# Expert stage of a token-routing kernel: row numbers made ahead of the new pick, X two steps sooner

## The chip, the cores and the metric

One NeuronCore of one Trainium2 chip runs the whole program in one launch. The metric is the device time of one execution in microseconds, smaller is better. The engines are TensorE (PE, with its weight loads as PEld), VectorE (DVE), ScalarE (ACT), GpSimd (POOL) and SyncE (SP); each runs its own list of instructions in order and waits on semaphores for the others.

## The reference

Three layers follow each other: a linear attention with decay, a dense feed-forward layer, and a mixture of 8 experts with a fixed capacity. The change concerns the last alone.

```python
def _attn_ref(r, k, v, w, u):                 # 4 batches, 8 heads, 768 steps, 48 features
    for t in range(S):
        y[:, :, t] = einsum('bhd,bhde->bhe', rt, state + (u * kt) outer vt)
        state = wt[:, :, :, None] * state + kt outer vt

def _moe_ref(x, w_in, w_out):                 # 3072 x 384, 384 x 2048, 2048 x 384
    h = x @ w_in
    return (h * np.tanh(softplus(h))) @ w_out

def _moe2_ref(x, w_gate, w1, w2):             # 8 experts, each 384 x 1024 and 1024 x 384
    cap = N // E                              # 384 tokens for each expert
    for idx in np.argsort(-(x @ w_gate).flatten()):
        tok, e = int(idx) // E, int(idx) % E  # best pair first; skip taken tokens, full experts
        ...
    for e in range(E):
        out[assigned == e] = np.maximum(x[assigned == e] @ w1[e], 0.0) @ w2[e]
```

## The kernel before

The first stage (attention and dense layer) runs over 12 blocks of 256 tokens. Its end leaves 3072 rows of 384 numbers in DRAM (`x2_d`) and the scores `L` of 24 x 8 for each of the 128 partitions in SBUF.

The second stage has to find out which 384 tokens go to which expert. It does so in rounds r = 0 to 6, called searches here: each names the expert that fills up first and the threshold above which its tokens lie, by six steps of a search with 32 thresholds at once. One step is: VectorE compares all keys with the 32 limits (`cmp`), TensorE counts in 24 small matmuls (`counts`), VectorE marks which experts are full (`filled`), TensorE sums the marks over the limits in one small matmul (`maxima`), VectorE makes the next limits (`next_step`). After the sixth step VectorE chooses expert and members (`choose`), TensorE makes their running numbers (`ranks`), VectorE takes the chosen tokens out and picks each remaining token's best expert anew (`pick_expert`, `one_hot_expert`, `start_search`).

The running numbers have to become a list of token numbers by slot: VectorE splits each number into digits and makes one-hot rows of them (`digits`, `numbered`, `one_hot_low`), TensorE multiplies them (unit I), VectorE masks the result (`id_blocks`), TensorE spreads it (unit J), VectorE sums it to `ids` (`token_ids`). With `ids` GpSimd gathers the expert's rows from DRAM (`rows_in`).

The expert's own work on TensorE is cut into units. X is nine transposes of the gathered rows, whose result ScalarE rounds to fp16 (`xgT_hi`) and VectorE reduces to a remainder (`low_xg`). H0 to H7 are nine matmuls each of 384 columns with the first weights; ScalarE rounds each, VectorE makes its remainder (`low_h`). Y0 to Y7 are nine matmuls each with the second weights, added up in three banks. H0 waits for both parts of X; Yf waits for both parts of Hf. After Y7, ScalarE copies the rows out of the banks.

TensorE's list is written out by hand. In every search there are 13 places for units, written in `PLACES`: place A of step t lies between `counts` and `maxima` of that step, place B behind `maxima`, and place C behind `ranks`. `units(r, where, do)` says which expert is meant; expert p is the one that search p chose. Before, I, J, X, H0 to H3 and Y0 of search r belong to expert r-1, the others to expert r-2. VectorE's list is written out in the loop over searches, with `low_h` and `low_xg` put between the search's own instructions. While nothing is there for TensorE in search 1, products that nobody reads are run (`idle_products`). Behind the last search the same places go on without counts and maxima until expert 7 is done.

Of the kernel before, what the change touches and what calls it, by code (L numbers as in the profile page):

```python
# [14 lines left out]
B, H, S, D = 4, 8, 768, 48  # L15
# [7 lines left out]
NT = N // P  # L23
# [37 lines left out]
def moe_chain(nc, wt_d, kt_d, rt_d, r_d, k_d, v_d, u_d, win_d, wout_d, wg_d, wot_d, w1_d, w2_d, out_d):  # L61
# [4 lines left out]
    with ctx:  # L66
# [223 lines left out]
        def split_out(n):  # L290
# [4 lines left out]

        PLACES = {("A", 0): ["Y1"], ("B", 0): ["H4"], ("A", 1): ["I", "Y2"], ("B", 1): ["J", "H5"],
# [3 lines left out]
        YOUNG = ("X", "H0", "H1", "H2", "Y0", "H3")  # L300
        ORDER = [(c, t) for t in range(NSTEP) for c in "AB"] + [("C", 0)]
# [4 lines left out]
        def units(r, where, do):  # L306
            for u in PLACES[where]:
                p = r - 1 if u in YOUNG + ("I", "J") else r - 2
                if 0 <= p < E:
                    do(p, u[0], int(u[1:] or 0))  # L310
# [112 lines left out]
        def _(pe):  # L423
# [358 lines left out]
            for r in range(E - 1):  # L782
                if r == 1:
                    idle_products(16)
                for t in range(NSTEP):
                    counts(r, t)
                    units(r, ("A", t), unit)
                    if r == 0:
                        sums(NI - 1, SUMS["B", t], slice(0, 3))
                    maxima(r, t)  # L790
                    if r == 1 and t < 4:
                        idle_products(6)
                    units(r, ("B", t), unit)
                    if r == 0:
                        sums(NI - 1, SUMS["B", t], slice(3, None))
                ranks(r)
                units(r, ("C", 0), unit)
            ranks(E - 1)
# [193 lines left out]
        def _(dve):  # L992
# [135 lines left out]

            def pick_expert(js=slice(0, NT), fill_a=None, fill_b=None):
                n = js.stop - js.start  # L1130
                link(V.tensor_reduce(val[:, js], L3[:, js, :], AX.X, ALU.max))
                if fill_a:
                    fill_a()
                link(V.tensor_tensor(less[:, js, :], L3[:, js, :], over_e(val[:, js]), ALU.is_lt))
                link(V.tensor_tensor(tmp3[:, js, :], less[:, js, :], over_j(eighths[:, :], n), ALU.add))
                if fill_b:
                    fill_b()
                link(V.tensor_reduce(pick[:, js], tmp3[:, js, :], AX.X, ALU.min))
# [301 lines left out]
            for t in range(2, NSTEP):  # L1440
                link(V.tensor_scalar(grid[t][:, :], iota_t[:, :], wid[:, t:t + 1], None, ALU.mult))

            for r in range(E - 1):
                new, old = r - 1, r - 2
                if r >= 1:
                    one_hot_low()
                filled(r, 0)
                low_h(old, 3)
                next_step(r, 0)
                filled(r, 1)  # L1450
                if r >= 1:
                    id_blocks(r - 1)
                low_h(old, 4)
                next_step(r, 1)
                if r >= 1:
                    token_ids(r - 1)
                filled(r, 2)
                low_h(old, 5)
                next_step(r, 2)
                filled(r, 3)  # L1460
                low_h(old, 6)
                next_step(r, 3)
                filled(r, 4)
                low_h(old, 7)
                next_step(r, 4)
                low_xg(new)
                filled(r, 5)
                choose(r)
                pick_expert(slice(0, NT), lambda: low_h(new, 0), lambda: low_h(new, 1))
                if r < E - 2:  # L1470
                    one_hot_expert()
                else:
                    weight_row(E - 1, pick[:, 0:1])
                take_slots(r)
                leave()
                if r < E - 2:
                    start_search()
                    digits()
                    numbered()
                    low_h(new, 2)  # L1480
            did(V.memset(mem[:, NT:2 * NT], 0.0))
            link(V.tensor_scalar(mem[:, 0:NT], gone[:, :], 0.0, None, ALU.is_equal))
            prefixes()
            low_h(E - 3, 2)
            digits()
            numbered()
            low_h(E - 3, 3)
            one_hot_low()
            low_h(E - 3, 4)
            id_blocks(E - 2)  # L1490
            token_ids(E - 2)
            low_h(E - 3, 5)
            take_slots(E - 1)
            digits()
            numbered()
            low_h(E - 3, 6)
            one_hot_low()
            low_h(E - 3, 7)
            low_xg(E - 2)
            for f in range(6):  # L1500
                low_h(E - 2, f)
                if f == 4:
                    id_blocks(E - 1)
                    token_ids(E - 1)
            low_h(E - 2, 6)
# [181 lines left out]
```

## Time and profile before

| what | value |
|---|---|
| median of 3 runs | 799.06 us (798.05 to 803.17) |
| the profiled execution | 798.34 us, its span 796.6 us |
| first stage, about | 0 to 513 us |
| searches 0 and 1, about | 513 to 565 us |
| searches 2 to 6 | 565 to 720.7 us |
| what follows search 6 | 720.7 to 796.6 us |
| busy over the span | PE 97%, PEld 72%, DVE 79%, ACT 53%, POOL 37% |

The profile is of one execution; its time is told beside its span, and 1.74 us lie outside the span. Times in the rows below are microseconds from the start of the span. "start us, us" are start and length of an instruction or of a row of equal ones (x24 is 24 of them); what stands in brackets is how long the engine was idle before it and who released it. A row of matmuls is pipelined, so that the next one may begin up to 0.16 us before the printed end. In a row of windows the bounds and the length come first, then the busy us of each engine with its number of instructions (PE, PEld, DVE, ACT, POOL, or PE alone), the granted clock of TensorE as a share of 2.4 GHz, the busy share of the DMA engines and GB/s.

### The profile page before, as it was taken

What the parts mean: (1) busy time and instruction counts of PE and PEld (TensorE: products, weight loads), DVE (VectorE), ACT (ScalarE), POOL (GpSimd) and SP (SyncE); (2) the same over time, 40 slices, a digit from 0 to 9 for tenths busy, and PEclk for the clock granted to TensorE, in tenths of its full rate; (3) what the DMA queues carried; (4) which work ended last, traced back from release to release, by engine and by line L of the source; (5) the groups of instructions that cost most, each with busy time, mean ns of one, the idle gap of its engine ahead of it and who ended that gap; (6) DMA issues with size and microseconds to landing.
All of it is one profiled execution on the core that took longest, in us unless ns stands there. A gap on an engine that the chain in (4) does not pass through costs nothing.

```text
span 796.6 us, 17145 instructions
## 1 busy us (share of the span) xinstructions
PE 769.7 (97%) x6810; PEld 577.1 (72%) x6810; DVE 628.6 (79%) x1081; ACT 425.1 (53%) x703; POOL 292.7 (37%) x244
## 2 busy tenths in 40 slices
PE   8899999999999999999999999987999999999994
PEld 8888878787878787878787877655565665666662
DVE  8969999999998999998999985877776767766220
ACT  2478759595968595868686779410121221222221
POOL 4424482627272727272726350011221231222311
PEclk9999999999999999999999999995999999999998
DMA  9962266464656464655464347114423415415500
GB/s 306 377 210 64 78 201 245 144 237 142 233 187 213 151 230 159 212 210 196 170 208 174 117 154 248 61 53 157 172 90 148 188 61 189 187 44 207 218 31 30
DMA packets 47791, 133.49 MB, mean 168 GB/s; under 512 B 5344, under 2 KB 19808, under 8 KB 45664
## 3 DMA queue, kind: packets, MB, share of 16 engines
q1 hardware_dynamic: 38880, 93.07, 33.7%
q0 software_dynamic: 5376, 34.61, 11.8%
q10 hardware_dynamic: 3456, 4.72, 1.7%
q8 instruction: 54, 0.88, 0.4%
q14 instruction: 25, 0.20, 0.1%
HBM read 97.78 MB, written 34.60 MB: 166 GB/s over the span
## 4 chain that ended last, share of the span: by engine, by line
PE 83%; DVE 10%; issue 2%; DMA 2%; ACT 2%; POOL 0%; SPq 0%; DVEq 0%
PE bank L425 80%; DVE cmp L1316 2%; DMA stage<-in_moe_w_out 1%; DVE g_lo L1416 1%; ACT t_sb L807 1%; PE bank L730 1%; PE bank L450 1%; PE bank L511 1%; DVE inv L1008 1%; DMA k_tok<-in_k 1%; DVE t_sb L1395 1%; DVE rdec L1023 0%; DVE t_sb L1388 0%; DVE t_sb L1391 0%; DVE thr L1333 0%
## 5 line engine op out<-in xcount | busy, mean ns | idle before, releaser
L425 PE MATMUL bank<-x_hi,win_hi 128*128 128x256 f16 (+1 forms) x588 | 158.8, 272 | 1.6 <-DVE h_sb L1080 0.9
L425 PE MATMUL bank<-x_lo,win_hi 128*128 128x256 f16 (+1 forms) x588 | 158.7, 272 | 0.0
L425 PE MATMUL bank<-x_hi,win_lo 128*128 128x256 f16 (+1 forms) x588 | 158.7, 272 | 0.0
L1547 POOL TENSOR_TENSOR g_lo<-t_sb,g_hi 128x512 f16<-128x512 f32 x88 | 122.3, 1420 | 47.0 <-ACT g_hi L807 47.0
L425 PE MATMUL bank<-wout_hi,g_hi 128*128 128x392 f16 (+1 forms) x416 | 129.0, 317 | 0.0
L425 PE MATMUL bank<-wout_lo,g_hi 128*128 128x392 f16 (+1 forms) x416 | 128.8, 316 | 0.0
L425 PE MATMUL bank<-wout_hi,g_lo 128*128 128x392 f16 (+1 forms) x416 | 128.7, 316 | 0.0
L807 ACT ACTIVATE g_lo<-bank 128x384 f16<-128x384 f32 x64 | 31.4, 490 | 144.1 <-PE bank L425 124.7
L1530 POOL TENSOR_TENSOR dv<-v_tok,dot 128x384 f32<-128x384 f32 x24 | 29.8, 1240 | 186.7 <-DVE dot L1038 186.7
L807 ACT ACTIVATE g_hi<-t_sb 128x512 f16<-128x512 f32 x96 | 56.5, 624 | 54.6 <-PE bank L425 54.4
L1087 DVE TENSOR_TENSOR t_sb<-t_sb,h_sb 128x512 f32<-128x512 f32 x96 | 83.0, 913 | 2.0 <-ACT t_sb L807 1.4
L1008 DVE RECIPROCAL inv<-cum 128x256 f32<-128x256 f32 x48 | 82.1, 1733 | 0.7
L807 ACT ACTIVATE t_sb<-h_sb 128x512 f32<-128x512 f32 x96 | 59.8, 623 | 37.5 <-DVE h_sb L1080 37.5
L807 ACT ACTIVATE t_sb<-t_sb,half 128x512 f32<-128x512 f32 x96 | 68.6, 715 | 0.1
L425 PEld LDWEIGHTS bank<-x_hi,win_hi 128*128 128x128 f16 x588 | 61.0, 104 | 9.7 <-issue 1.0
L1416 DVE SCALAR_TENSOR_TENSOR g_lo<-bank,g_lo 128x384 f16<-128x384 f32 x64 | 35.1, 549 | 40.5 <-ACT g_lo L807 34.1
L425 PEld LDWEIGHTS bank<-x_hi,win_lo 128*128 128x128 f16 x588 | 60.9, 104 | 6.0
L425 PEld LDWEIGHTS bank<-x_lo,win_hi 128*128 128x128 f16 x588 | 59.2, 101 | 6.3
L807 ACT ACTIVATE h_sb<-bank 128x512 f32<-128x512 f32 (+1 forms) x72 | 38.5, 556 | 43.4 <-PE bank L425 41.6
L807 ACT ACTIVATE t_sb<-t_sb,half_pi 128x512 f32<-128x512 f32 x96 | 60.8, 710 | 0.1
L1633 POOL DMA_INDIRECT out<-h_sb,ids x24 | 23.6, 983 | 98.1 <-ACT h_sb L807 93.3
L425 PEld LDWEIGHTS bank<-wout_hi,g_lo 128*128 128x128 f16 x416 | 42.9, 105 | 22.6
(184 smaller groups left out, 1593.7 us busy)
## 6 DMA issues: line engine op xcount, KB each, us to landing
stage<-in_moe_w SPq DMA_DIRECT2D x22, 768.0 KB, 6.5
w_split<-stage SPq DMA_DIRECT2D x22, 768.0 KB, 4.5
fold_w<-in_moe_w SPq DMA_DIRECT2D x10, 768.0 KB, 8.9
w_split<-fold_w SPq DMA_DIRECT2D x10, 768.0 KB, 7.6
wt<-in_w_turned SPq DMA_DIRECT2D x24, 258.0 KB, 2.8
kt<-in_k_turned SPq DMA_DIRECT2D x24, 256.0 KB, 2.6
rt<-in_r_turned SPq DMA_DIRECT2D x24, 256.0 KB, 2.8
r_tok<-in_r SPq DMA_DIRECT2D x24, 192.0 KB, 6.0
```

Of the source, the lines that this page charges most:

```text
L425: return nc.tensor.matmul(*a, **k)
L450: last = nc.tensor.transpose(T2[:, q * P:(q + 1) * P], kdiv[n % CH][:, q, :], ident[:, :])
L511: last = nc.tensor.transpose(Y[:, k3 * P:(k3 + 1) * P], x_tok[c][:, k3 * P:(k3 + 1) * P], ident[:, :])
L730: last = nc.tensor.transpose(bank[3 + k3][:, m * P:(m + 1) * P], xg[m][:, k3 * P:(k3 + 1) * P], ident[:, :])
L807: return nc.scalar.activation(out, in_, f, **k)
L1008: V.reciprocal(inv[:, qs, :], cum[n % CH][:, qs, 1:PW]).then_inc(s["inv"], 1)
L1087: V.tensor_tensor(t, t, h_sb[:, j * GW:(j + 1) * GW], ALU.mult).then_inc(s["g"], 1)
L1316: V.tensor_tensor(cmp[:, :, :], over_t(x[:, :], NTHR), limits[:, :].rearrange("p (o i) -> p o i", o=1).to_broadcast([P, NT, NTHR]), ALU.is ...
L1416: V.scalar_tensor_tensor(h_lo[f % 3][:, :], bank[3 + f % 3][:, 0:CAP], 0.0, h_hi[f % 3][:, :], ALU.max, ALU.subtract).then_inc(s["hlo"], 1)
L1530: G.tensor_tensor(dv[:, :, :], v_tok[c][:, :, :], dot[:, :].rearrange("p (h o) -> p h o", o=1).to_broadcast([P, H, D]), ALU.mult).then_inc ...
L1547: G.tensor_tensor(g_lo[:, j * GW:(j + 1) * GW], t_sb[:, j * GW:(j + 1) * GW], g_hi[:, j * GW:(j + 1) * GW], ALU.subtract).then_inc(s["glo" ...
L1633: G.indirect_dma_start(out_d, bass.IndirectOffsetOnAxis(ap=ids[p % 3][:, m:m + 1], axis=0), y_sb[m][:, :], None).then_inc(s["yout"], 16)
```

## The change

`PLACES` is written anew. X stands two steps earlier (place B of step 2 instead of step 4). Places A of steps 2 and 3 are empty, H0 and H1 follow in B of step 3, and from there one unit stands in each place until C, which holds seven: H4, Y2, I, H5, J, Y3, H6. I and J there are of the expert that this very search has chosen. Only Y4, H7, Y5, Y6 and Y7 are left for the next search.

VectorE's list follows. After `choose` it makes the row numbers at once (`take_slots`, `digits`, `numbered`, `one_hot_low`, `id_blocks`), and only then the new pick, and `token_ids` ahead of `start_search`. `low_xg` moves from behind step 4's `next_step` to behind step 2's. The idle products of search 1 move: 28 now stand behind `ranks` of search 0, around I and J of expert 0, and 12 in search 1 (before 40 in search 1). The number and the shape of all other instructions stay as they are.

```diff
--- before.py
+++ after.py
@@ -293,11 +293,11 @@
 
 
 
-        PLACES = {("A", 0): ["Y1"], ("B", 0): ["H4"], ("A", 1): ["I", "Y2"], ("B", 1): ["J", "H5"],
-                  ("A", 2): ["Y3"], ("B", 2): ["H6"], ("A", 3): ["Y4"], ("B", 3): ["H7"],
-                  ("A", 4): ["Y5"], ("B", 4): ["X", "Y6"], ("A", 5): ["Y7"],
-                  ("B", 5): ["H0", "H1"], ("C", 0): ["H2", "Y0", "H3"]}
-        YOUNG = ("X", "H0", "H1", "H2", "Y0", "H3")
+        PLACES = {("A", 0): ["Y4"], ("B", 0): ["H7", "Y5"], ("A", 1): ["Y6"], ("B", 1): ["Y7"],
+                  ("A", 2): [], ("B", 2): ["X"], ("A", 3): [], ("B", 3): ["H0", "H1"],
+                  ("A", 4): ["Y0"], ("B", 4): ["H2"], ("A", 5): ["Y1"], ("B", 5): ["H3"],
+                  ("C", 0): ["H4", "Y2", "I", "H5", "J", "Y3", "H6"]}
+        OLDER = ("Y4", "H7", "Y5", "Y6", "Y7")
         ORDER = [(c, t) for t in range(NSTEP) for c in "AB"] + [("C", 0)]
 
 
@@ -305,7 +305,7 @@
 
         def units(r, where, do):
             for u in PLACES[where]:
-                p = r - 1 if u in YOUNG + ("I", "J") else r - 2
+                p = r - 2 if u in OLDER else r if u in ("I", "J") else r - 1
                 if 0 <= p < E:
                     do(p, u[0], int(u[1:] or 0))
 
@@ -780,21 +780,26 @@
                     mm(bank[2][:, 0:TOK], x_hi[0][:, 0, 0:P], x_hi[0][:, 1, :], start=True, stop=True)
 
             for r in range(E - 1):
-                if r == 1:
-                    idle_products(16)
                 for t in range(NSTEP):
                     counts(r, t)
                     units(r, ("A", t), unit)
                     if r == 0:
                         sums(NI - 1, SUMS["B", t], slice(0, 3))
                     maxima(r, t)
-                    if r == 1 and t < 4:
+                    if r == 1 and t < 2:
                         idle_products(6)
                     units(r, ("B", t), unit)
                     if r == 0:
                         sums(NI - 1, SUMS["B", t], slice(3, None))
                 ranks(r)
-                units(r, ("C", 0), unit)
+                if r == 0:
+                    idle_products(8)
+                    unit(0, "I", 0)
+                    idle_products(8)
+                    unit(0, "J", 0)
+                    idle_products(12)
+                else:
+                    units(r, ("C", 0), unit)
             ranks(E - 1)
             for r in range(E - 1, E + 2):
                 for where in ORDER:
@@ -1126,15 +1131,11 @@
             def over_t(x, n):
                 return x.rearrange("p (j o) -> p j o", o=1).to_broadcast([P, NT, n])
 
-            def pick_expert(js=slice(0, NT), fill_a=None, fill_b=None):
+            def pick_expert(js=slice(0, NT)):
                 n = js.stop - js.start
                 link(V.tensor_reduce(val[:, js], L3[:, js, :], AX.X, ALU.max))
-                if fill_a:
-                    fill_a()
                 link(V.tensor_tensor(less[:, js, :], L3[:, js, :], over_e(val[:, js]), ALU.is_lt))
                 link(V.tensor_tensor(tmp3[:, js, :], less[:, js, :], over_j(eighths[:, :], n), ALU.add))
-                if fill_b:
-                    fill_b()
                 link(V.tensor_reduce(pick[:, js], tmp3[:, js, :], AX.X, ALU.min))
 
             def one_hot_expert(js=slice(0, NT)):
@@ -1440,68 +1441,61 @@
             for t in range(2, NSTEP):
                 link(V.tensor_scalar(grid[t][:, :], iota_t[:, :], wid[:, t:t + 1], None, ALU.mult))
 
+            def steps_of(r):
+
+                filled(r, 0)
+                next_step(r, 0)
+                low_h(r - 2, 7)
+                filled(r, 1)
+                next_step(r, 1)
+                filled(r, 2)
+                next_step(r, 2)
+                low_xg(r - 1)
+                filled(r, 3)
+                next_step(r, 3)
+                low_h(r - 1, 0)
+                filled(r, 4)
+                low_h(r - 1, 1)
+                next_step(r, 4)
+                filled(r, 5)
+                low_h(r - 1, 2)
+                choose(r)
+
+            def row_numbers():
+                digits()
+                numbered()
+                one_hot_low()
+
             for r in range(E - 1):
-                new, old = r - 1, r - 2
-                if r >= 1:
-                    one_hot_low()
-                filled(r, 0)
-                low_h(old, 3)
-                next_step(r, 0)
-                filled(r, 1)
-                if r >= 1:
-                    id_blocks(r - 1)
-                low_h(old, 4)
-                next_step(r, 1)
-                if r >= 1:
-                    token_ids(r - 1)
-                filled(r, 2)
-                low_h(old, 5)
-                next_step(r, 2)
-                filled(r, 3)
-                low_h(old, 6)
-                next_step(r, 3)
-                filled(r, 4)
-                low_h(old, 7)
-                next_step(r, 4)
-                low_xg(new)
-                filled(r, 5)
-                choose(r)
-                pick_expert(slice(0, NT), lambda: low_h(new, 0), lambda: low_h(new, 1))
+                steps_of(r)
+                low_h(r - 1, 3)
+                take_slots(r)
+                row_numbers()
+                low_h(r - 1, 4)
+                id_blocks(r)
+                pick_expert(slice(0, NT))
                 if r < E - 2:
                     one_hot_expert()
                 else:
                     weight_row(E - 1, pick[:, 0:1])
-                take_slots(r)
+                token_ids(r)
                 leave()
                 if r < E - 2:
                     start_search()
-                    digits()
-                    numbered()
-                    low_h(new, 2)
+                low_h(r - 1, 5)
+                low_h(r - 1, 6)
             did(V.memset(mem[:, NT:2 * NT], 0.0))
             link(V.tensor_scalar(mem[:, 0:NT], gone[:, :], 0.0, None, ALU.is_equal))
             prefixes()
-            low_h(E - 3, 2)
-            digits()
-            numbered()
-            low_h(E - 3, 3)
-            one_hot_low()
-            low_h(E - 3, 4)
-            id_blocks(E - 2)
-            token_ids(E - 2)
-            low_h(E - 3, 5)
             take_slots(E - 1)
-            digits()
-            numbered()
-            low_h(E - 3, 6)
-            one_hot_low()
             low_h(E - 3, 7)
+            row_numbers()
             low_xg(E - 2)
-            for f in range(6):
+            for f in range(5):
                 low_h(E - 2, f)
-                if f == 4:
-                    id_blocks(E - 1)
-                    token_ids(E - 1)
+            id_blocks(E - 1)
+            low_h(E - 2, 5)
+            token_ids(E - 1)
             low_h(E - 2, 6)
             low_h(E - 2, 7)
             low_xg(E - 1)
```

## Rows read from the trace of the kernel before

**Rows 1.** The page: span and chain that ended last, by engine.

```profile
span 796.6 us, 17145 instructions
...
PE 83%; DVE 10%; issue 2%; DMA 2%; ACT 2%; POOL 0%; SPq 0%; DVEq 0%
```

**Rows 2.** Windows: the whole of search 3 (busy us of each engine, clock, DMA).

```profile
595.96:627.16 31.20, 30.92 (x313) 18.85 (x312) 22.87 (x73) 6.43 (x14) 7.76 (x8) 1.00 0.38 139
```

**Rows 3.** Timeline of TensorE, two steps of search 5 (start us, length us).

```profile
666.83 0.76 PE L425 MATMUL bank<-oh,cmp 128*32 128x8 bf16 x24
...
669.09 0.17 PE L425 MATMUL bank<-full,rest_b 32*128 32x8 bf16 x1
...
670.80 0.76 PE L425 MATMUL bank<-oh,cmp 128*32 128x8 bf16 x24
```

**Rows 4.** Timeline of TensorE: three units of expert 6, one more, and the last products.

```profile
737.96 4.55 PE L425 MATMUL bank<-g_hi,win_hi 128*128 128x384 f16 x27
...
742.35 1.63 PE L425 MATMUL bank<-win_lo,g_lo 128*128 128x384 f16 x9
...
782.96 4.55 PE L425 MATMUL bank<-wout_lo,g_lo 128*128 128x384 f16 x27 [1.27 <-DVE g_lo L1416]
```

**Rows 5.** Timelines of TensorE, ScalarE and VectorE, one X in search 4.

```profile
645.83 0.17 PE L425 MATMUL bank<-full,rest_b 32*128 32x8 bf16 x1
...
646.58 1.25 ACT L807 ACTIVATE g_hi<-bank 128x384 f16<-128x384 f32 x3 [2.45 <-PE bank L730]
...
647.64 1.48 DVE L1424 SCALAR_TENSOR_TENSOR g_hi<-bank,g_hi 128x384 f16<-128x384 f32 x3
...
649.32 0.15 DVE L1326 TENSOR_SCALAR full<-bank 32x8 bf16<-32x8 f32 x1 [0.20 <-PE bank L425]
```

**Rows 6.** Timelines of TensorE and VectorE, end of search 0.

```profile
530.13 0.17 PE L425 MATMUL bank<-full,ones_b 32*128 32x8 bf16 x1
...
532.17 0.26 DVE L1354 TENSOR_TENSOR_SCAN before<-mem,zeros 128x47 bf16<-128x47 bf16 x1
...
533.10 0.35 DVE L1131 TENSOR_REDUCE val<-L 128x24 f32<-128x192 f32 x1
...
536.49 0.17 DVE L1384 TENSOR_SCALAR high<-slot 128x24 f32<-128x24 f32 x1
...
537.78 0.95 DVE L1395 TENSOR_TENSOR t_sb<-low,iota_lo 128x768 f16<-128x768 f32 x1
```

**Rows 7.** Timelines of TensorE and GpSimd, search 1 and the start of search 2.

```profile
536.72 0.74 PE L425 MATMUL bank<-oh,cmp 128*32 128x8 bf16 x24 [2.27 <-DVE cmp L1316]
...
540.57 0.80 PE L425 MATMUL bank<-oh,cmp 128*32 128x8 bf16 x24 [0.78 <-DVE cmp L1316]
...
543.41 0.80 PE L425 MATMUL bank<-oh,cmp 128*32 128x8 bf16 x24
...
544.56 0.18 PE L425 MATMUL bank<-full,rest_b 32*128 32x8 bf16 x1 [0.35 <-DVE full L1326]
...
547.36 0.95 POOL L1626 DMA_INDIRECT h_sb<-x_rows,ids  x1 [0.30 <-issue]
...
551.72 2.18 PE L730 MATMUL bank<-ident,h_sb 128*128 128x128 f32 x9
...
555.25 5.51 PE L425 MATMUL bank<-g_hi,win_hi 128*128 128x384 f16 x18
...
565.13 0.76 PE L425 MATMUL bank<-oh,cmp 128*32 128x8 bf16 x24
```

**Rows 8.** Windows: TensorE and its granted clock where it falls and rises.

```profile
71.20:74.90 3.70, 2.79 (x27) 1.00 0.21 69
...
75.50:76.00 0.50, 0.50 (x5) 0.50 0.96 299
...
534.46:539.00 4.54, 0.89 (x26) 1.00 0.77 271
...
555.20:560.60 5.40, 5.40 (x19) 2.62 (x20) 4.00 (x17) 0.49 (x1) 2.02 (x2) 0.54 0.19 41
```

## The prediction

> **What bounds the kernel now.** I read the chain that ended last first. It is TensorE's for 83% of the span [rows 1], so a wait of another engine counts only where TensorE stands still for it. Then the windows, one for each search: TensorE is busy for 30.92 of 31.20 us at the full clock, VectorE for 22.87 [rows 2]. The reader is to see that in the searches 2 to 6 TensorE is full and VectorE is not. Nothing is left to win there by giving TensorE its work earlier; the only room is in search 1, where it runs products for nobody, and the only danger is that a search, once full, gets holes.
>
> Then the timeline of TensorE, for the prices. Three units of the experts take 742.35 - 737.96 = 4.39 us, one 1.46 [rows 4]. A step with one unit in each place takes 670.80 - 666.83 = 3.97, of which 2.26 lie between the start of `counts` and `maxima` and 1.71 behind it [rows 3]. The 1.71 are also what VectorE needs from `maxima` to new compared keys (in search 1 too, see below), so the unit in place B covers a chain as long as itself. Without units a step takes 543.41 - 540.57 = 2.84, and `maxima` begins 544.56 - 543.41 = 1.15 after `counts` [rows 7]. What matters most: these two chains, TensorE to VectorE and back, are in the step itself. A place that is empty doesn't shorten the search by its unit, it uncovers the chain, and the unit is run elsewhere at its full price.
>
> **The change part by part.** I count a search from its `maxima` of step 5, called M, and price each place.
>
> *Behind M, H3 alone.* `ranks` waits for the scan that ends choosing: 532.17 + 0.26 against `maxima` at 530.13, 2.30, and with the hand-over 2.35 [rows 6]. Before, H0 and H1 (2.93 us) cover it. One unit ends at M + 1.57, so 0.8 us stand open.
>
> *C, with I.* H4 and Y2 end at M + 5.35. I needs `one_hot_low`. VectorE is through with `choose` at 533.10 - 530.13 = 2.97. From there: `low_h` 3 0.47, `take_slots` 0.23 (before it stood further back at the same length), then from `high` to the end of the one-hot rows 537.78 + 0.95 - 536.49 = 2.24 [rows 6]: M + 5.9, with the hand-over 6.0. TensorE stands 0.65 us. H5, J, Y3 and H6 go to M + 10.6. Beside them VectorE makes `low_h` 4, `id_blocks`, the pick, `token_ids` and the first keys: 0.5 + 0.2 + 2.0 + 0.6 + 0.4 + 0.9, to M + 10.4. That just fits; 0.3 us more on VectorE would be 0.3 more on TensorE. From M to the next search: 10.7.
>
> *Step 0:* three units, 0.69 + 1.46 + 2.93 and 0.35 of changes, 5.4. *Step 1:* 3.97. *Step 2:* no unit in A, X in B. X lasts 1.0 us, less than the chain, so the step is that of search 1, 2.85.
>
> *Step 3, the hole.* `low_xg` now stands behind `next_step` of step 2 and ahead of `filled` of step 3. Before, the same order stood one place from here with Y units beside it. There `maxima` is at 645.83, ScalarE has rounded X at 647.83, VectorE is through with `low_xg` at 649.12 and `filled` begins at 649.32, 3.49 behind `maxima` [rows 5]. In step 2 `next_step` is one small instruction longer (0.25). `maxima` of step 3, and H0 behind it, thus come 3.95 us behind `maxima` of step 2, and TensorE has X and one `counts` to do, 1.8 us. Two us stand open. Queued behind that `maxima` is all the rest of the search. Step 3 from `counts`: 2.25 to `maxima`, then H0 and H1, 3.15: 5.4. *Step 4:* 3.97. *Step 5* to M: 2.26.
>
> Sum of a search: 10.7 + 5.4 + 3.97 + 2.85 + 5.4 + 3.97 + 2.26 = 34.5 us, where it was 31.2: +3.3 in each of five.
>
> TensorE runs its units in the order written, so nothing that stands behind a waiting `maxima` slips into its hole.
>
> *The start.* After search 0, VectorE ends `choose` at 533.1. Row numbers take 0.23 + 0.43 + 2.24 - 0.43 to 535.6, I and `id_blocks` to 536.1, the pick to 538.0, `token_ids` to 538.6, keys and compare to 540.0. `counts` of search 1 begins at 540.1, where it was 536.72: 3.4 us later, and nothing covers it. In return step 0 and 1 of search 1 carry no row numbers. Two steps of 2.87 bring step 2 to 545.8, its `maxima` and X to 546.9 (X was at 551.72), H0 to 550.9 (was 555.25) [rows 7]. The gain is 4.35 us.
>
> X there needs the rows. GpSimd issued the third gather until 548.31, 3.4 us ahead of X, which didn't wait for it [rows 7]. The new `ids` let it end at about 542.5, 4.4 ahead of X. But now the gathers run while the first weights still arrive. Bounds: nothing, or all of the gain (X back at 551.7), 4.8 us. I take nothing, since the distance grows. In later searches `ids` lie over 10 us ahead of X, and GpSimd's rows out come far ahead of the next weights: nothing. The 28 idle products lie in the wait for VectorE: nothing.
>
> *From H0 on.* H0 and H1 at the half clock 5.4 as before (560.60 - 555.20) [rows 8], to 556.3; step 4 to 560.3; step 5 and C, 12.95, to 573.2. Search 2 began at 565.13, but six units (8.8 us) fewer were done by then: at this point the change is 0.7 us ahead. Four searches of 34.5 and one of 34.4 lead to 745.6.
>
> *The end.* `ranks` of the last expert stands ahead of Y4. Its members are now made behind `low_h` 6, which waits for H6: the scan ends about 1.6 us after TensorE arrives. 747.2. Five units, 7.3. Then X with H0 right behind it: rounding and remainder end 2.8 us after X starts (0.65 + three of 0.5 + the last remainder 0.6, from rows 5 without the other work), X is 1.0, so 1.8 stand open, twice; before, Y6 and Y7 covered this. 754.5 + 2.8 + 16 units and I, J 23.6 + 2.8 + 16 units 23.4 + the last wait 1.3 [rows 4] = 808.4. From the last product's start-of-next to the end of the span it was 796.6 - 787.35 = 9.25: 817.6. With the 1.74 outside the span, 819.3.
>
> *The clock.* Twice in these rows it falls after TensorE ran only narrow or no matmuls: after 71.2 to 74.9 with narrow products of the weight fold and a wait, and after 534.46 with `counts` and idle time; at 75.5 it is at half, and it stays at half until 560 at the later place [rows 8]. Each new search has such a stretch: from Y7 in step 1 to H0 in step 3 there are 0.1 + 2.85 + 2.26 + 0.1 = 5.3 us with two `counts`, two `maxima` and nine transposes. It is longer than the 3.7 us at 71.2. So I expect falls to 1.2 GHz, and a price of H0 and H1 at half: 5.4 - 2.93 = 2.4 us [rows 8]. Bounds: 0 and 5 x 2.4 = 12. What the transposes count for, no row shows; I take three falls in five, 7.2.
>
> 819.3 + 7.2 = 826.5. The median of the runs lay 0.7 above the profiled execution. I forecast **827 us**.
>
> **The rivals.** *Holes without falls.* The transposes keep the clock up. For it: they fill 1.0 of the 5.3 us. Then 820 with the median's 0.7, and down to 811 if the holes are a half smaller than worked out (VectorE's two chains are measured, their overlap isn't).
>
> *Falls in every search.* The Trainium skill ("TensorE: Matmul & The Clock Gate", section "HAM oscillation") says that a loop whose every pass has a long enough hole pays the fall in every pass. As a mechanism here: the hole is the same in each search, so five falls at 2.4, or at up to 3.5 if the half clock outlasts H1: 832 to 838. The trace has only single falls.
>
> *Faster (the other side).* The start wins 4.35 and the two added steps of counting behind H0 cost 2 x 0.9; 2.5 are left. If the holes of a search came to under 0.5 us, the kernel would be faster, 796.6 at best. Place: step 3, `maxima` behind `low_xg`. For it speaks only that VectorE has 8.3 us to spare in a search [rows 2]; against it that these stand elsewhere.
>
> *It does nothing.* The gathers come too late for the new X, the search stretches, and the end is set by the same sum of products: 799 to 803. All holes would have to be covered too.
>
> **How the numbers follow.** Forecast (two to four falls, 821 to 832) 0.5; holes without falls, 811 to 821, 0.25; falls in every search, 832 to 838, 0.12; smaller holes, 803 to 811, 0.05; does nothing 0.03; faster 0.05. The range 811 to 836 leaves out under 0.2. About 1% is what a measurement here tells from no change. Faster by over 1%: half of the faster case, 0.03; within 1% (791 to 807): 0.07; slower 0.9.
>
> **What the new profile would show.** Searches 2 to 6 of about 34.5 us, more with falls; in each an idle TensorE of about 2 us ahead of `maxima` of step 3, ended by VectorE's `full`; 0.8 ahead of `ranks`; 0.65 ahead of I. X of expert 0 near 547, H0 near 551. `counts` of search 1 near 540.1. The granted clock under 1 around H0 in some searches. Wrong would make me: a VectorE that finishes `low_xg` before `next_step` is due, transposes that hold the clock, or rows that come late in search 1.

## The result, and the profile after

The changed kernel takes 840.31 us (837.96 to 842.25), the kernel before 799.28: 1.0502 times as long, with a 95% interval of 1.0474 to 1.0531. The forecast was 827 with a range to 836. The direction was right; the size was 13 us short, and 4 outside the range.

The profiled execution took 842.25 us, its span 840.5. The page of the changed kernel, the rows that answer to [rows 1]:

```profile
span 840.5 us, 17145 instructions
...
PE 82%; DVE 10%; another core or an unknown queue 2%; DMA 2%; issue 1%; SPq 1%; ACT 1%; POOL 0%; DVEq 0%
```

The same number of instructions lies in 43.9 us more. Its windows of search 2, to set beside [rows 2]:

```profile
577.36:614.91 37.55, 32.89 (x313) 19.43 (x312) 23.37 (x73) 6.43 (x14) 8.32 (x9) 0.95 0.30 117
```

The search was 31.20 us and is 37.55. TensorE is busy for 32.89 us with the same 313 matmuls that took 30.92, because its clock was granted at 0.95, and it stands for 4.7 us, where it stood 0.3. So there are two losses: 4.4 us more of standing and 2.0 us more of busy time for the same matmuls. The timeline of TensorE says where (changed kernel, search 2, the steps' own instructions and those that waited):

```profile
577.36 0.76 PE L425 MATMUL bank<-oh,cmp 128*32 128x8 bf16 x24
...
580.43 0.17 PE L425 MATMUL bank<-full,rest_b 32*128 32x8 bf16 x1 [0.75 <-DVE full L1327]
...
588.62 0.17 PE L425 MATMUL bank<-full,rest_b 32*128 32x8 bf16 x1 [0.32 <-DVE full L1327]
588.72 1.21 PE L730 MATMUL bank<-ident,h_sb 128*128 128x128 f32 x9
590.33 0.76 PE L425 MATMUL bank<-oh,cmp 128*32 128x8 bf16 x24 [0.40 <-DVE cmp L1317]
592.97 0.17 PE L425 MATMUL bank<-full,rest_b 32*128 32x8 bf16 x1 [1.88 <-DVE full L1327]
593.08 4.78 PE L425 MATMUL bank<-g_hi,wout_hi 128*128 128x384 f16 x18
597.79 0.76 PE L425 MATMUL bank<-oh,cmp 128*32 128x8 bf16 x24
...
604.25 0.17 PE L425 MATMUL bank<-full,ones_b 32*128 32x8 bf16 x1
...
606.59 0.20 PE L425 MATMUL bank<-mem,rank_b 128*128 128x48 bf16 x1 [0.60 <-DVE before L1355]
...
610.25 0.32 PE L425 MATMUL bank<-t_sb 128*128 128x48 f16 x6 [0.50 <-DVE t_sb L1396]
...
614.91 0.76 PE L425 MATMUL bank<-oh,cmp 128*32 128x8 bf16 x24
```

The hole stands where it was put: 1.88 us ahead of `maxima` of step 3, and `ranks` and I wait 0.60 and 0.50. Two things are not as priced. From that `maxima` to the next `counts`, with H0 and H1 (x18), it is 597.79 - 592.97 = 4.82 us, where 3.15 was said, and this in all five searches, 1.7 each. And `maxima` of step 0 waits 0.75 for a `filled` that began late. Windows of TensorE around the hole of search 2 (changed kernel):

```profile
588.70:592.90 4.20, 1.99 (x34) 1.64 (x34) 3.37 (x9) 1.42 (x4) 3.09 (x3) 1.00 0.26 94
593.08:597.80 4.72, 4.72 (x20) 2.23 (x19) 2.30 (x6) 0.49 (x1) 0.00 (x0) 0.64 0.08 28
```

Through the hole the granted clock is still 1.00; behind it, with H0, it is 0.64, a mix of both levels. Such a drop of the granted clock is called a fall below. In this search the bill for it comes to the work behind the hole.

The late `filled`, timelines of VectorE and GpSimd, changed kernel, start of search 2:

```profile
580.22 0.15 DVE L1327 TENSOR_SCALAR full<-bank 32x8 bf16<-32x8 f32 x1 [1.67 <-remote]
```
```profile
578.42 0.94 POOL L1620 DMA_INDIRECT h_sb<-x_rows,ids  x1 [0.30 <-issue]
```

`counts` had ended at 578.1, VectorE was free since 578.6, and `filled` began at 580.22, 0.86 us behind the end of GpSimd's third gather. The profile names neither TensorE nor GpSimd as what ended the wait, but "remote", which is to say another core or an unknown queue. The change had put the gathers of an expert right across the first `counts` of the next search. In the kernel before they lay beside step 3 (there the third ended at 577.98), and in its trace `filled` came late there too, but a Y unit stood in front of `maxima` (kernel before, VectorE; the `counts` named in brackets had ended at 577.95):

```profile
578.97 0.15 DVE L1326 TENSOR_SCALAR full<-bank 32x8 bf16<-32x8 f32 x1 [1.43 <-PE bank L425]
```

The tail (changed kernel, timeline of TensorE):

```profile
766.87 0.20 PE L425 MATMUL bank<-mem,rank_b 128*128 128x48 bf16 x1 [1.56 <-DVE before L1355]
...
774.28 1.15 PE L730 MATMUL bank<-ident,h_sb 128*128 128x128 f32 x9
777.74 4.77 PE L425 MATMUL bank<-g_hi,win_hi 128*128 128x384 f16 x18 [2.31 <-ACT g_hi L812]
...
802.99 1.15 PE L730 MATMUL bank<-ident,h_sb 128*128 128x128 f32 x9
806.45 3.08 PE L425 MATMUL bank<-g_hi,wout_hi 128*128 128x384 f16 x18 [2.31 <-ACT g_hi L812]
```

and of ScalarE there:

```profile
774.48 1.25 ACT L812 ACTIVATE h_sb<-bank 128x384 f32<-128x384 f32 x3 [3.90 <-PE bank L425]
775.61 1.28 ACT L812 ACTIVATE g_hi<-bank 128x384 f16<-128x384 f32 x3
```

From X to H0 it is 3.46 us, twice, where 2.8 was said: ScalarE copies the rows that Y7 had just finished (1.25 us) ahead of rounding X. Behind the first X the clock fell once more (4.77 for 3.08), behind the second it didn't.

### The profile page after: what moved, and what is told of

Same layout as the page of the kernel before. It is cut to its first block, busy times and chain, and to the rows that moved or that the text cites. A ratio compares the mean times of both kernels' runs of the same rounds, so it can differ in the third digit from the quotient of the medians.

```text
span 840.5 us, 17145 instructions
## 1 busy us (share of the span) xinstructions
PE 786.7 (94%) x6810; PEld 582.4 (69%) x6810; DVE 630.4 (75%) x1081; ACT 425.1 (51%) x703; POOL 296.3 (35%) x244
## 4 chain that ended last, share of the span: by engine, by line
PE 82%; DVE 10%; another core or an unknown queue 2%; DMA 2%; issue 1%; SPq 1%; ACT 1%; POOL 0%; DVEq 0%
PE bank L425 80%; DVE cmp L1317 2%; DMA fold_w<-in_moe_w_out_turned 2%; DVE g_hi L1425 1%; PE bank L450 1%; DVE g_lo L1417 1%; PE bank L511 1%; DVE t_sb L1396 1%; SPq L321 0%; ACT g_lo L812 0%; DVE t_sb L1389 0%; DVE t_sb L1392 0%; DVE full L1327 0%; DVE most L1331 0%
## 5 line engine op out<-in xcount | busy, mean ns | idle before, releaser
L425 PE MATMUL bank<-x_hi,win_hi 128*128 128x256 f16 (+1 forms) x588 | 160.9, 276 | 0.6 <-DVE x_lo L1076 0.6
L425 PE MATMUL bank<-x_lo,win_hi 128*128 128x256 f16 (+1 forms) x588 | 160.9, 276 | 0.0
L425 PE MATMUL bank<-x_hi,win_lo 128*128 128x256 f16 (+1 forms) x588 | 160.8, 275 | 0.0
L425 PE MATMUL bank<-g_hi,win_hi 128*128 128x384 f16 x288 | 58.7, 358 | 2.3 <-ACT g_hi L812 2.3
```

The source lines that it names most:

```text
L425: return nc.tensor.matmul(*a, **k)
```

## The experiments

Ratios are to the kernel before on the same chip. Where kernels are compared by their traces, it matters that what comes ahead of the change, the first stage above all, ends at different times from one execution to the next: `ranks` of search 0 begins at 532.48 in the trace of before, 535.28 in that of after, and between 532.58 and 536.91 in the others, that of a repeat of the kernel before (799.44 us) at 535.78. So I compare stretches from there on, and "the first stage" below means all up to that point.

**The changed kernel again**, unchanged.

> The changed kernel once more, beside the others of this call. In its first trace filled came 1.0 us or more late in step 0 of each search and 0.4 late in step 3, 1.2 us a search; in the four experiments so far, those with filled in its old form too, it came late nowhere. Theory A (the lateness comes and goes with the run or the chip, whatever form filled has): 838 to 842 us if this trace shows it, 831 to 834 if not. Rival B (it belongs to this program, and the experiments removed it by what they changed): 840 us and late filled as in the first trace.

It took 835.1 us (832.72 to 836.5), 1.0454 [1.0418, 1.049]. Search 3 in its timeline of TensorE:

```profile
614.70 0.17 PE L425 MATMUL bank<-full,rest_b 32*128 32x8 bf16 x1
...
622.89 0.17 PE L425 MATMUL bank<-full,rest_b 32*128 32x8 bf16 x1 [0.32 <-DVE full L1327]
...
626.59 0.17 PE L425 MATMUL bank<-full,rest_b 32*128 32x8 bf16 x1 [1.23 <-DVE full L1327]
...
631.41 0.76 PE L425 MATMUL bank<-oh,cmp 128*32 128x8 bf16 x24
```

`maxima` of step 0 no longer waits, and that of step 3 waits 1.23 instead of 1.88. The five searches take 749.39 - 568.42 = 180.97 us, 36.19 each (it was 37.55). In each H0 and H1 are slow: from `maxima` to `counts` it is 4.46, 4.82, 5.98, 4.51 and 4.82 us, where the kernels below without a fall have 3.14. That is 8.9 us in all. So the falls belong to the kernel; the late `filled` is in one of its two traces. The four executions of this repeat took 832.72 to 836.5, the first four 837.96 to 842.25.

**The kernel before again**, for the same comparison.

> The kernel before once more, for its trace on this chip: filled of step 3 was 1.03 us late in its first trace, hidden behind the unit in place A. Theory A (comes and goes): it is late or not as in e5; the search stays 31.2 us either way and the time 797 to 800. Rival B (belongs to the program): late as before.

799.44 us, a single run; searches of 31.2 us as in [rows 2], so nothing of the two losses. `filled` of step 3, 1.0 us late in each of the searches 2 to 6 of the first trace, is late in none here.

**Products for nobody in the holes** of searches 2 to 6. The text of each step stays, TensorE only isn't left without work (`hole_products(n)` is n products of 256 columns into a bank that nobody reads).

```diff
                     units(r, ("A", t), unit)
+                    if r >= 2 and t in (2, 3):
+                        hole_products({2: 2, 3: 14}[t])
                     ...
                     maxima(r, t)
                     ...
                     units(r, ("B", t), unit)
+                    if r >= 2 and t == 2:
+                        hole_products(3)
```

> The changed kernel with products that nobody reads in the holes of searches 2 to 6: 2 behind counts of step 2, 3 behind X, 14 behind counts of step 3 (2.1 us of matmuls in 2.6 us of standing). Theory A (the holes cost twice, once as standing time and once by the fall of the clock that they bring): the clock stays at 2.4 GHz in searches 2 to 6, H0 and H1 take 2.9 us instead of 4.7, a search 35.8 us instead of 37.55, the kernel 831.5 us against 840.3. Rival B (the falls have nothing to do with what TensorE runs in the hole): falls as before, 840 us or, with the products in the way, up to 843.

826.35 us, 1.0352 [1.0326, 1.0378]: nearly 9 us less than the changed kernel's repeat, though nothing was moved and TensorE got 19 matmuls more in each search. Its timeline of TensorE in search 3:

```profile
621.90 0.17 PE L425 MATMUL bank<-full,rest_b 32*128 32x8 bf16 x1
...
624.30 1.70 PE L425 MATMUL bank<-x_hi 128*128 128x256 f16 x14
625.94 0.17 PE L425 MATMUL bank<-full,rest_b 32*128 32x8 bf16 x1
626.05 3.10 PE L425 MATMUL bank<-g_hi,win_hi 128*128 128x384 f16 x18
```

From `maxima` to `maxima` it is 4.04 (forecast 3.95, in the repeat 3.70), so the hole's time is still paid in full, and 0.3 us on top; but H0 and H1 are back at 3.10. A search takes 646.21 - 611.46 = 34.75 us (35.8 was expected, from the trace with the late `filled`); the forecast without falls was 34.5. This splits the loss of a search in the repeat: 1.8 of clock, and 36.19 - 1.8 - 31.2 = 3.2 of standing, in the hole and ahead of `ranks` and I. The theory of the falls holds, the rival, that the products change nothing, doesn't. But not all of the 9 us is theirs: five searches give 5 x (36.19 - 34.75) = 7.2, and 1.6 come from search 1, which has no added products and in which H0 and H1 took 1.5 us less in this execution.

**Products in every thin stretch**, the same with r >= 1, six more behind `maxima` of search 1's steps 0 and 1, and twelve behind X in the tail.

> The changed kernel with products for nobody in every thin stretch: as before in the holes of searches 2 to 6, and now in search 1 and behind X in the tail. Theory A (the holes alone, without any fall): no granted clock under 0.9 between 540 us and the end, searches of 34.6, span 819 to 823, 2 to 6 us less than with products in the searches alone (826.3). Rival B (the tail's stretch is lengthened as much as its clock gains, or the fall only moves): 825 to 829.

822.23 us, 1.0309 [1.0282, 1.0335], span 820.9. Behind X in the tail (timeline of TensorE):

```profile
756.34 1.15 PE L730 MATMUL bank<-ident,h_sb 128*128 128x128 f32 x9
757.32 1.47 PE L425 MATMUL bank<-x_hi 128*128 128x256 f16 x12
759.80 3.08 PE L425 MATMUL bank<-g_hi,win_hi 128*128 128x384 f16 x18 [1.00 <-ACT g_hi L822]
```

The distance from X to H0 is again 3.46, H0 and H1 are at 3.08 instead of 4.77: 1.7 us. Against the products in the searches alone the span is 4.7 less, but 3.8 of that is a first stage that ended earlier (533.09 for 536.91), 1.5 the tail, and search 1 lost 0.7. There the expectation failed: in spite of the added products the granted clock was 0.66 from 540 to 546 and 0.81 from 546 to 553.3; it is 1.00 only from there on, in every search and in the tail. So this is the price of the holes of searches 2 to 6 and of the tail without falls: with `ranks` of search 0 at 533.09, 820.9 - 533.09 = 287.8 us are left; the forecast's own sum, with a half clock in search 1 as well, was 817.6 - 532.48 = 285.1.

**Another form of `filled`**, two tensors instead of a tensor and a number, in case the form was what GpSimd held up.

```diff
-V.tensor_scalar(full[:, :], bank[6][0:NTHR, 0:E], float(CAP), None, ALU.is_ge)
+V.tensor_tensor(full[:, :], bank[6][0:NTHR, 0:E], caps[:, :], ALU.is_ge)
```

> The changed kernel with filled as a tensor_tensor against a tile of 384s instead of a tensor_scalar with an immediate; same result. The trace shows filled beginning 1.0 us or more late whenever GpSimd issues indirect DMAs around it (step 0: third gather; step 3: third rows out). Theory A (this form of VectorE instruction is held up by GpSimd's issuing): filled follows counts and low_xg by 0.1 us, a search is 1.15 us shorter, the start 1.5, the kernel 833 us against 840.3. Rival B (the wait is for something else, a late count from TensorE or a transfer): filled is as late as before, 840 us.

832.66 us, 1.0432 [1.0414, 1.0449], as expected, and `filled` wasn't late. But it was not late in the repeat of the changed kernel with the old form either, and the two intervals overlap. The reason that I gave falls: with either form it can come in time.

**Row numbers early, X where it was.** One part of the change on the kernel before: VectorE's order of the change, I and J of the new expert in C (C: H2, Y0, I, H3, J), and the products for nobody around I and J of expert 0 as in the change; all other units in their old places.

> One part of the change alone: the kernel before with I and J of the new expert in place C and the row numbers made ahead of the new pick, X and all H and Y left where they were. Theory A (making the row numbers first puts 3 us of VectorE work ahead of the next keys, and C with its three units no longer covers it): C lasts 10.4 us instead of 7.5, a search 34.2 instead of 31.2, search 1 starts 3.4 us later, the kernel 817 to 820 us. Rival B (the price of the change is X's place and the empty places alone): 799 to 803 us.

820.77 us, 1.0296 [1.0271, 1.0321], 0.8 above the interval of theory A. Its timeline of TensorE at the start of search 4:

```profile
637.42 0.19 PE L425 MATMUL bank<-blocks,copies 128*128 128x48 f16 x1
640.19 0.74 PE L425 MATMUL bank<-oh,cmp 128*32 128x8 bf16 x24 [2.59 <-DVE cmp L1321]
640.86 2.74 PE L425 MATMUL bank<-win_lo,g_lo 128*128 128x384 f16 x9
643.53 0.18 PE L425 MATMUL bank<-full,rest_b 32*128 32x8 bf16 x1
```

With only H2, Y0 and H3 beside I and J in C the longer chain of VectorE is not covered: `counts` of the next search waits 2.59 us for `cmp`, and the Y unit behind it takes 643.53 - 640.86 = 2.67 instead of 1.46, with the clock granted at 0.57 there. Again both parts of the bill, at another place; the fall comes in three of the five searches. That is what the seven units in C were needed for.

**X one step sooner, the row numbers where they were.** The order of before, all units from X on two places earlier (X in B of step 3).

> The kernel before with X one step sooner and every place still filled: the order of units is kept and shifted by two places (X and Y6 in B of step 3, Y7, H0, H1, then H2 and Y0 in B of step 5, three units in C), row numbers where they were. Theory A (with no place empty an earlier X wins what it wins at the start): X of expert 0 at 549, H0 at 552.5 instead of 555.25, searches 2 to 6 still 31.2 us, the kernel 796.5 us against 799.3. Rival B (an earlier X meets its rows: the third gather is issued until just ahead of it, so X waits up to 1 us in each search): 800 to 804 us.

804.83 us, 1.0086 [1.007, 1.0103], where the rival had said 800 to 804. Its timeline of TensorE, in search 1 and in search 3:

```profile
550.84 2.18 PE L730 MATMUL bank<-ident,h_sb 128*128 128x128 f32 x9 [3.17 <-DMA h_sb<-x_rows,ids]
...
614.60 1.20 PE L730 MATMUL bank<-ident,h_sb 128*128 128x128 f32 x9 [0.51 <-DMA h_sb<-x_rows,ids]
```

X now arrives ahead of its rows and gains nothing. With the row numbers where they were, one step sooner is already too soon: it costs 0.8 us a search (31.97 on average for 31.2).

**The places of the change, the row numbers where they were.** The other part alone: X in B of step 2 and empty places as changed, but I and J of the previous expert in steps 0 and 1, and VectorE's row numbers behind the new pick.

> The kernel after with X as early as there, but with the row numbers where the kernel before had them (after the new pick, I and J in steps 0 and 1). Theory A (the two parts belong together): ids come to stand only in step 2, X of step 2 waits for the gather, in every search TensorE stands still ahead of X by about 5 us instead of the hole of 2 behind it; TensorE doesn't wait for I in C, so a search is 36 to 38 us at the full clock, and the whole is 835 to 848, as slow as the changed kernel or slower. Rival B (the row numbers are the dearer half, X alone is cheap): X waits under 1 us, as it did one place earlier, and the whole stays under 825.

869.52 us, 1.0884 [1.0863, 1.0904], far above my interval. Its timeline of TensorE, search 3:

```profile
630.36 0.17 PE L425 MATMUL bank<-full,rest_b 32*128 32x8 bf16 x1 [0.39 <-DVE full L1322]
636.21 2.18 PE L730 MATMUL bank<-ident,h_sb 128*128 128x128 f32 x9 [5.67 <-DMA h_sb<-x_rows,ids]
...
639.62 0.18 PE L425 MATMUL bank<-full,rest_b 32*128 32x8 bf16 x1 [0.50 <-DVE full L1322]
...
644.28 0.76 PE L425 MATMUL bank<-oh,cmp 128*32 128x8 bf16 x24
```

X waits 5.67 us for its rows (I had said 5). A search takes 653.10 - 612.23 = 40.87 us, where I had 36 to 38 at the full clock. I had left the clock out once more: X takes 2.18 for 1.20, and from `maxima` to `counts` behind it it is 4.66 for 3.14, together 2.5. What is left is 38.4. The tail, from `ranks` of search 6 on, takes 93.8 us for the repeat's 83.6, and X waits 5.9 and 5.1 us there as well. So the two parts of the change do belong together: X this early needs the early row numbers, and the early row numbers need the long C. Together (835 to 840 us) they are cheaper than X's part alone (870), and dearer than the row numbers alone (821) or no change (798).

**The hole filled with a unit of its own.** Y7 of the older expert goes from step 1 behind X, into A of step 3; Y5 and Y6 each move one place back to close the gap.

```diff
-("A", 0): ["Y4"], ("B", 0): ["H7", "Y5"], ("A", 1): ["Y6"], ("B", 1): ["Y7"],
-("A", 2): [], ("B", 2): ["X"], ("A", 3): [], ("B", 3): ["H0", "H1"],
+("A", 0): ["Y4"], ("B", 0): ["H7"], ("A", 1): ["Y5"], ("B", 1): ["Y6"],
+("A", 2): [], ("B", 2): ["X"], ("A", 3): ["Y7"], ("B", 3): ["H0", "H1"],
```

> The changed kernel with the units behind H7 moved by one place: B of step 0 has H7 alone, then Y5, Y6, nothing, X, and Y7 in place A of step 3, where TensorE stands for low_xg. Theory A (a unit costs its 1.46 us only where no chain of VectorE hides it; in the hole it is free): a search is 1.4 us shorter than in e5, the end behind search 6 some 4 us shorter (Y7 between X and H0, twice), the clock falls in fewer searches: 11 to 20 us less than e5. Rival B (the holes aren't what costs; TensorE's sum of work is): as e5 within 3 us.

812.22 us, 1.0183 [1.0149, 1.0218], 23 less than the changed kernel's repeat. Its timeline of TensorE, search 4:

```profile
650.12 0.17 PE L425 MATMUL bank<-full,rest_b 32*128 32x8 bf16 x1 [0.32 <-DVE full L1327]
...
652.52 1.64 PE L425 MATMUL bank<-win_lo,g_lo 128*128 128x384 f16 x9
654.09 0.17 PE L425 MATMUL bank<-full,rest_b 32*128 32x8 bf16 x1
654.19 3.10 PE L425 MATMUL bank<-g_hi,wout_hi 128*128 128x384 f16 x18
```

The distance from `maxima` to `maxima` is 3.97 (forecast 3.95, in the repeat 3.70), but 1.46 us of it now carry a unit, and no fall follows in any of the five searches. A search takes 33.27 us; 5 x (36.19 - 33.27) = 14.6. In the tail from `ranks` of search 6 to the end it is 77.5 instead of 83.6, since Y7 now covers part of the way from X to H0 and the clock doesn't fall there; the remaining 2.1 us are a first stage that ended earlier, so some 21 of the 23 are the move's. Against before's 31.2 there are still 2 us a search: X's empty step 2, and the waits of `ranks` and I.

**The kernel before with more products for nobody in search 1** (34 instead of 16 behind `ranks`, 14 instead of 6 behind each of the first four `maxima`, 6 in step 4), to see what the half clock there is worth [rows 8]. Twice, with 12 and 7 runs.

> The kernel before with more products for nobody in search 1: 34 instead of 16 behind ranks, 14 instead of 6 in place B of steps 0 to 3, and 6 in step 4, all in time that TensorE stood idle. Theory A (a fall of the clock is brought by what TensorE doesn't run, and is worth what H0, H1 and X lose at 1.2 GHz): the clock stays at 2.4 GHz to the end of search 1, H0 and H1 take 2.9 us instead of 5.4 and X 1.2 instead of 2.2, the kernel 795.5 us against 798.5. Rival B (the clock falls anyway, and products at the half clock are in the way of counts): 800 us.

> The kernel before with more products for nobody in search 1, run again since the first time did not tell it apart. Theory A: the clock stays full from search 1's start to H0 and it is 1 to 3 us faster than the kernel before (795.5 to 797). Rival B: the ratio's interval holds 1 again at more runs, what the clock gains in search 1 is not seen in the whole.

796.69 us, 0.999 [0.9967, 1.0013], and 795.87 us, 0.9973 [0.9949, 0.9996]. Windows of search 1 in the first and in the second trace, each from 534 to 553:

```profile
534.00:553.00 19.00, 16.22 (x250) 13.50 (x248) 15.29 (x48) 2.16 (x4) 4.97 (x5) 1.00 0.57 212
```
```profile
534.00:553.00 19.00, 16.74 (x211) 13.05 (x210) 13.67 (x43) 1.28 (x1) 5.29 (x5) 0.82 0.58 214
```

In the first the clock stays at 1.00 and `ranks` of search 1 comes at 556.93 instead of 560.6. In the second it fell although the same products were there:

```profile
539.92 0.17 PE L425 MATMUL bank<-full,rest_b 32*128 32x8 bf16 x1 [1.39 <-DVE full L1328]
540.03 2.66 PE L425 MATMUL bank<-x_hi 128*128 128x256 f16 x14
```

What TensorE did before the fall doesn't tell the two apart. In both it waits 0.30 us ahead of `counts` of step 0 and then 1.4 ahead of `maxima` (1.39 here, 1.40 in the first trace), yet the 14 products behind it take 2.66 us here and 1.70 in the first. What decided is not shown. The execution with the fall took 798.21, where 12 of the 19 took 795 to 797.3. So 2 us are there to be had in most executions, and at most 0.3% is left of them in the median: the first interval holds 1, the second ends at 0.9996. It is the only version here with a median below that of the kernel before, and the two can barely be told apart.

## Why the prediction was right in direction and short in size

*The holes: right.* The forecast had 34.5 us for a search at the full clock. The repeat of the changed kernel takes 36.19 with falls of 8.9 / 5 = 1.8 on average, so 34.4 without; the kernels with products take 34.75. The single waits were 1.56 ahead of the last `ranks` (said 1.6), 0.60 (0.8), 0.50 (0.65) and 1.23 to 1.88 (2; from `maxima` to `maxima` 3.70 and 4.35, said 3.95). `counts` of search 1 came 7.55 us behind `ranks` (540.1 - 532.48 = 7.6 said). The rows in search 1, priced between nothing and 4.8 and taken as nothing, made X wait 0.53 in the repeat.

*Step 0 and GpSimd's queue, the step that failed.* The forecast counted nothing on GpSimd's queue but whether the rows came in time, and had `maxima` follow `counts` by 2.26 us in step 0 wherever the gathers lay. In the trace of after VectorE's `filled` came late beside them: in search 1 X came 551.21 - 542.83 = 8.38 us behind `counts`, in the repeat 7.35; in each of five searches 0.82 in step 0 (3.07 from `counts` to `maxima` for 2.25) and 0.65 in step 3. Together 1.0 + 5 x 1.47 = 8.4 us against the repeat, the largest missing term, and the one that took the result out of the range: the repeat, without it, took 835.1, just inside. It could have been read before: the first trace of the kernel before had it in searches 2 to 6, 1.0 us behind its third gather, with a Y unit as cover, and the change moved the gathers to a place where nothing covers it.

*"The clock": the mechanism right, the term too small.* I took three falls in five at 2.4, 7.2 us. There were five in five, in both traces of the changed kernel, at 1.7 and 1.8, and a sixth of 1.7 in the tail, which was in no bound although I had worked out the same standing time there: in the repeat 8.9 + 1.7 = 10.6 us, 3.4 more. The reason for three was that no row showed what the transposes count for. The rival "falls in every search" had the mechanism right. The Trainium skill ("TensorE: Matmul & The Clock Gate", section "HAM oscillation") tells of a loop in which the clock falls again in every pass. The trace agrees on that, five of five, though the wait in the page's loop is one for a transfer and here no single wait ahead of these falls was over 1.88 us. The products in the holes show it by experiment, 7.2 us back in five searches for added work.

*A smaller missing term.* ScalarE's copies of the older expert's rows ahead of X's rounding in the tail: 2 x 0.65 = 1.3. I had taken X's row "without the other work".

*The sum.* Repeat: 817.6 + 2.8 first stage + 8.9 + 1.7 falls + 1.3 copies = 832.3, span 833.0. After has 8.4 more for `filled` and 5 x (4.82 - 3.14) = 8.4 instead of 8.9 for the falls: 840.2, span 840.5. This is the sum of the profiled execution, the slowest of the four. The first stage's 2.8 us are no part of the change, since the repeat of the kernel before shows 3.3 as well.

*Open.* What holds `filled` back is not settled. In the searches 2 to 6 of the first trace of each kernel it begins 0.84 to 1.01 us behind the end of the third gather (in step 3 of after 0.34 to 0.39 behind the last rows out), and in these searches of the 11 later traces it comes in time, in those of the same two kernels too. So neither the gathers' place nor the form of the instruction is enough to bring it, and what differed between the first two traces and the later ones, the chip or something else, no run separates. Nor is it shown that this is all that separates 840.3 from 835.1, since only one execution of each was traced.

## What to carry to other kernels

A place that you empty on a full engine costs twice: the chain that it uncovers, and a slower clock for the work right behind it, in every pass of the loop; look for each place where the standing time recurs, the tail as well, and count all of them. When a unit moves earlier, leave an independent unit behind it to cover its rounding: one unit put there gave back more than half of the loss. Look in the trace of before for waits that only a neighbouring unit covers, such as the late `filled`, since a new order can uncover them. Two moves that need each other have to be priced apart too, each alone, for that shows which wait the other one pays for.

## What the runs showed of the hardware that was not expected

- Work for nobody pays: 19 more matmuls in each of five searches made these searches 7.2 us faster together, since the stretch behind them took 3.14 us instead of 4.46 to 5.98.
- In the changed kernel's searches 2 to 6 and its tail, up to the last product, TensorE never stood longer than 2.31 us at a stretch (in a search 0.32, 0.40 and 1.88 between narrow matmuls and transposes) and lost its clock all the same; and the same X with the same 2.31 us behind it cost the clock at 774 and not at 803; in the repeat it was again the first of the two and not the second (4.76 and 3.08).
- `ranks` of search 0, with the same code ahead of it throughout, began between 532.48 and 536.91 in 13 traces. A difference of 4 us between two spans is nothing before that is looked at.
